# Input parts of later token pairs made ahead, and weights rounded a period ahead, in a fused attention and mixture-of-experts kernel

## The chip, the cores and the metric

The kernel runs on one core of one Trainium2 chip. The metric is the device time of one launch in microseconds; 0.2% of it is 3.75 us. The engines are called PE (TensorE), DVE (VectorE), ACT (ScalarE), POOL (GpSimd) and SP (SyncE, which issues the DMAs).

## The reference

Four batches of eight attention heads over 576 positions, with a learned bias on the scores, give x of 2304 tokens by 512 features. Then every token goes through all eight experts, and the outputs are added with weights from a gate that is normalised over rows and columns eight times:

```python
logits = x @ w_gate
logits = logits - logits.max()
P = np.exp(logits)
for _ in range(8):
    P /= P.sum(1, keepdims=True) + 1e-09
    P /= P.sum(0, keepdims=True) + 1e-09
    P *= N / E
out = np.zeros((N, D), dtype=np.float32)
for e in range(E):
    h = np.maximum(x @ w1[e], 0.0)
    ye = h @ w2[e]
    out += P[:, e:e + 1] * ye
```

with N = 2304 tokens, D = 512, E = 8 experts and F = 1024 hidden units each.

## The kernel before

The first 345 us are attention; from there on the kernel is the expert stage. Tokens are taken in three pairs of blocks of 384 (`TILE_PAIRS` = 3, numbered p = 0 to 2). For each pair the loop goes over 32 periods: eight experts, four pairs of 128 hidden units each. So g, the period, runs from 0 to 95, and p = g // 32. The three pairs use the same weights, loaded again for each.

In a period PE does two things. First **seven products**: x @ w1 for two blocks of tokens and two of hidden units is a 2 by 2 block product, done in seven block products instead of eight (sums and differences of blocks on both sides). Each factor is kept as a rounded high part and the rest, its low part; a product is high by high, low by high and high by low, over two halves of the depth: six matmuls of 384 columns, 42 in all. Then **six tiles**: the second layer of the period before, h @ w2, six matmuls of 512 columns for each of six tiles of 128 tokens, 36 in all. 78 matmuls are one period.

What the other engines do for it in a period, each in the order of its own queue:

- ACT copies the first product out of PSUM (`keep_first`, p1_copy), later the third (`keep_corner`), rounds four blocks of h (`round_hidden`), and rounds the weights of the next period in three parts (`round_weights`: part 0 is raw blocks, 768 wide; part 1 the sums, 1024; part 2 is w2, 1024).
- DVE makes u2, u3 and three corners from the products (`combine`), and h_lo, the low parts of h (`split_hidden`, four). After an expert's last period it adds the six tiles to the output (`add_tile`). In periods 2 to 8 it also does the gate's normalisation; its column totals are small matmuls between PE's tiles.
- POOL makes the low parts of the weights (`split_weights`, three) and the weight sums two periods ahead (`sum_weights`, four). In periods 4 to 7 of a pair it makes the four sums of the next pair's blocks (`sum_factor`), over raw blocks of x that are no longer needed.
- SP loads the weights of a later period when both buffers of the stage allow it.

Everything is ordered by semaphores. PE's product 2 waits for p1_copy, product 3 for u2, product 4 for the corner copy, product 5 for u3, product 6 for the first corner. The weights w1 lie in two buffers, w2 in three. The third part of `round_weights` waits for `h_used`, which counts the periods whose tiles PE has done.

**At the start of a pair** the seven x factors have to be rounded (ACT, `round_factor`, into `x_hi`) and split (`split_factor`, into `x_lo`). There is one `x_hi` and one `x_lo` per factor, so a factor of the new pair can be made only when the last product of the old pair that reads it is done. Factors 0 and 1 and 4 are split on DVE and 2, 3, 5 and 6 on POOL, around the end of the pair's last period and in the first of the new one. In that first period PE doesn't do seven products and then six tiles, but mixes them:

```python
APART = ((), (0, 1), (), (2, 3), (), (4,), (5,))
TOGETHER = ((), (), (), (), (), (), tuple(range(TJ)))
```

Of the kernel before, what the change touches and what calls it, by code (L numbers as in the profile page):

```python
# [13 lines left out]
P = 128  # L14
# [33 lines left out]
APART = ((), (0, 1), (), (2, 3), (), (4,), (5,))  # L48
TOGETHER = ((), (), (), (), (), (), tuple(range(TJ)))
ON_GPSIMD = (2, 3, 5, 6)  # L50
# [34 lines left out]
def bass_attention_moe(nc, qk, v, bias_w, gate_w, expert_w, log_table, inv_psi, identity, pair_select, out):  # L85
    with ExitStack() as ctx:
# [24 lines left out]

        def first_weights(i):
            return [sb(f"w1_{part}{i}", [P, NP, BLOCK], F32R) for part in ("hi", "lo")]
# [16 lines left out]
        x = sb("x", [P, DC, N])  # L130
# [26 lines left out]
        logits_t = sb("logits_t", [P, 2, T])  # L157
# [4 lines left out]
        x_lo_first = sb("x_lo_first", [P, EARLY, 2, T], F32R)  # L162
        p1_copy = sb("p1_copy", [P, T])
        x_lo_rest = sb("x_lo_rest", [P, NP - EARLY, 2, T], F32R)
# [43 lines left out]
        x_split_late = sem("x_split_late")  # L208
# [59 lines left out]
        def x_block(p, half, part):  # L268

            return x[:, 2 * half:2 * half + 2, (2 * p + part) * T:(2 * p + part) * T + T]  # L270

        def x_sum(p, i):
# [4 lines left out]
            return x_block(p - 1, i % 2, i // 2)  # L277

        def x_factor(p, k):

            return (x_block(p, 0, 0), x_sum(p, 1), x_block(p, 1, 0), x_sum(p, 2), x_sum(p, 0), x_sum(p, 3),
                    x_block(p, 1, 1))[k]
# [17 lines left out]
        def tiles_after(g, k):  # L300

            return (APART if 0 < g < ALL and g % PERIODS == 0 else TOGETHER)[k]

        def x_low(k):
            return x_lo_first[:, k] if k < EARLY else x_lo_rest[:, k - EARLY]

        def splits_before(p, k):

            late = [j for j in ON_GPSIMD if j < k]
            if p == 0:  # L310
                return k, 0
            return NP + (NP - len(ON_GPSIMD)) * (p - 1) + k - len(late), len(ON_GPSIMD) * (p - 1) + len(late)

# [119 lines left out]
        def _(pe):  # L433
# [159 lines left out]
            def product(g, k):  # L593
# [3 lines left out]
                if g % PERIODS == 0:  # L597
                    on_vector, on_gpsimd = splits_before(p, k + 1)
                    if p > 0 and k in ON_GPSIMD:
                        pe.wait_ge(x_split_late, on_gpsimd)  # L600
                    else:
                        pe.wait_ge(x_split, on_vector)
# [25 lines left out]
                for c in range(2):  # L628
                    f = slice(c * P, c * P + P)
                    pe.matmul(dst, hi[:, w, f], x_hi[:, k, c, :], start=fresh and c == 0, stop=False,  # L630
                              skip_group_check=not fresh)
                    pe.matmul(dst, hi[:, w, f], x_low(k)[:, c, :], start=False, stop=False,  # L632
                              skip_group_check=not fresh)
                    mm = pe.matmul(dst, lo[:, w, f], x_hi[:, k, c, :], start=False, stop=c == 1,  # L634
# [89 lines left out]
            for g in range(ALL + 1):  # L724
                for k in range(NP):
# [4 lines left out]
                    if g > 0:  # L730
# [8 lines left out]
        def _(act):  # L739
# [77 lines left out]
            def round_weights(g, i):  # L817
# [14 lines left out]
            def round_factor(p, k):  # L832

                if p == 0:
                    act.wait_ge(scores_ready, 2 * (LAST - QC))
                    act.wait_ge(split_done, 2 * X_PIECES)
                    act.wait_ge(scaled, PIECES_0)
                else:
                    act.wait_ge(product_done, NP * (PERIODS * p - 1) + k + 1)
                needed = (0, 2, 0, 3, 1, 4, 0)[k]  # L840
                if needed:
                    act.wait_ge(x_summed, SUMS * p + needed)
                act.activation(x_hi[:, k], x_factor(p, k), ACT.Copy).then_inc(x_rounded, 1)
# [54 lines left out]
            for g in range(ALL):  # L898
                p, at = g // PERIODS, g % PERIODS
                more = g + 1 < ALL  # L900
                after = at == PERIODS - 1 and more
# [10 lines left out]
                if more:  # L912
                    round_weights(g + 1, 0)
# [3 lines left out]
                if after:  # L917
                    round_factor(p + 1, 0)
                if more:
                    round_weights(g + 1, 1)  # L920
                round_hidden(g, 1)
                if after:
                    round_factor(p + 1, 1)
                if more:
                    round_weights(g + 1, 2)
                round_hidden(g, 2)
                round_hidden(g, 3)
                if after:
                    for k in range(2, 5):
                        round_factor(p + 1, k)  # L930
# [3 lines left out]
        def _(dve):  # L934
# [116 lines left out]
            def split_factor(p, k):  # L1051
# [3 lines left out]
                dve.tensor_tensor(x_low(k), x_factor(p, k), x_hi[:, k].bitcast(F32),  # L1055
# [115 lines left out]
            for g in range(ALL):  # L1171
                p, at = g // PERIODS, g % PERIODS
                after = at == PERIODS - 1 and g + 1 < ALL
# [3 lines left out]
                if at == 0 and p > 0:  # L1177
                    split_factor(p, 4)
                    add_tile(g - 1, 0)
                dve.wait_ge(product_done, NP * g + 4)  # L1180
                combine(u3[:], product_bank(g, 1), p1_copy[:], ALU.add)
                if at == 0 and p > 0:
                    add_tile(g - 1, 1)
                    add_tile(g - 1, 2)
# [5 lines left out]
                split_hidden(g, 0)  # L1190
                if after:
                    split_factor(p + 1, 0)
# [3 lines left out]
                combine(corner[:, 3, :], product_bank(g, 0), u2[:], ALU.add)  # L1196
                split_hidden(g, 1)
# [3 lines left out]
                if at > 0:  # L1201
# [173 lines left out]
```

## Time and profile before

| | |
|---|---|
| median of three timed runs | 1874.88 us (1873.86 to 1876.94) |
| the profiled execution | 1876.01 us |
| its span, first to last instruction | 1874.2 us |
| PE busy | 1846.2 us, 99% |
| DVE, ACT, POOL busy | 1298.8, 809.3, 1139.4 us |
| mean granted clock of PE | 0.996 |

The span is the profiled execution without what lies before its first and behind its last instruction (1.8 us). PE is the engine that the others serve; the busy time of the others matters only where PE, or an engine that PE waits for, stands behind it. Matmuls overlap: one of 384 columns lasts 0.33 us and the next starts 0.17 us after it.

### The profile page before, as it was taken

Reading aid. Unit: us, or ns where it says so; the run is one execution under the profiler, and the core shown is the slowest. Engines: PE = TensorE matmul, PEld = TensorE weight load, DVE = VectorE, ACT = ScalarE, POOL = GpSimd, SP = SyncE. Lnnn points to the kernel's source line nnn. Section 1 sums busy time; section 2 is a strip of 40 time slices with the busy share of each in tenths; the row PEclk is TensorE's granted clock in tenths of the full one; section 3 lists DMA queues with packets and bytes.
Section 4 is the critical chain, followed back from the end, with each engine's and each line's share of the span. In section 5 each row is a group of like instructions: output and inputs, shape, how many; then the busy total and the mean of one; then the engine's idle time right before and its main releaser. Section 6 shows DMA issues by size and latency. Waiting matters only on the chain.

```text
span 1874.2 us, 28089 instructions
## 1 busy us (share of the span) xinstructions
PE 1846.2 (99%) x10255; PEld 1600.3 (85%) x10255; DVE 1298.8 (69%) x1838; ACT 809.3 (43%) x1410; POOL 1139.4 (61%) x728
## 2 busy tenths in 40 slices
PE   8999999999999999998999999999989999999999
PEld 4677777788899999997999999999889999999998
DVE  8877777778766666666666666666656666666664
ACT  8776777633333333333333333333433333333331
POOL 0223326467766666668687666666766666666662
PEclk9999999999999999999999999999999999999999
DMA  7753452011111111112112212111121111111110
GB/s 246 220 147 93 124 151 57 33 68 68 68 68 68 68 67 68 68 68 102 51 70 71 71 71 72 70 67 68 68 79 68 68 68 68 68 68 68 68 68 34
DMA packets 44163, 152.57 MB, mean 81 GB/s; under 512 B 9594, under 2 KB 18042, under 8 KB 29710
## 3 DMA queue, kind: packets, MB, share of 16 engines
q1 hardware_dynamic: 44046, 151.04, 24.7%
q8 instruction: 70, 1.15, 0.3%
q14 instruction: 47, 0.39, 0.1%
HBM read 135.69 MB, written 15.34 MB: 81 GB/s over the span
## 4 chain that ended last, share of the span: by engine, by line
PE 90%; DVE 4%; issue 1%; ACT 1%; POOL 0%; DVEq 0%; ACTq 0%; POOLq 0%
PE banks L663 13%; PE banks L664 13%; PE banks L662 13%; PE banks L630 12%; PE banks L634 12%; PE banks L632 12%; PE banks L541 4%; PE banks L502 3%; PE banks L484 3%; PE banks L485 2%; DVE h_lo L1145 2%; PE banks L567 1%; DVE routing L1113 0%; DVE x_lo_first L1055 0%; PE banks L512 0%
## 5 line engine op out<-in xcount | busy, mean ns | idle before, releaser
L1254 POOL TENSOR_TENSOR w_lo<-stage,w_hi 128x1024 fp32r<-128x1024 f32 (+1 forms) x288 | 689.8, 2421 | 460.8 <-ACT w_hi L830 459.6
L1145 DVE SCALAR_TENSOR_TENSOR h_lo<-corner,h_hi 128x384 fp32r<-128x384 f32 x384 | 648.8, 1718 | 0.0
L630 PE MATMUL banks<-x_hi,w_hi 128*128 128x384 f32 x1344 | 453.6, 338 | 13.1 <-DVE u L1139 6.5
L634 PE MATMUL banks<-x_hi,w_lo 128*128 128x384 f32 x1344 | 452.0, 336 | 0.0
L664 PE MATMUL banks<-w_hi,h_lo 128*128 128x512 f32 x1152 | 450.3, 391 | 0.0
L663 PE MATMUL banks<-w_lo,h_hi 128*128 128x512 f32 x1152 | 450.2, 391 | 0.0
L662 PE MATMUL banks<-w_hi,h_hi 128*128 128x512 f32 x1152 | 449.1, 390 | 0.0
L1139 DVE TENSOR_TENSOR u<-p_copy,banks 128x384 f32<-128x384 f32 x192 | 106.3, 554 | 423.0 <-PE banks L634 422.9
L860 ACT ACTIVATE p_copy<-banks 128x384 f32<-128x384 f32 x96 | 47.2, 492 | 710.7 <-PE banks L634 710.7
L830 ACT ACTIVATE w_hi<-stage 128x1024 fp32r<-128x1024 f32 (+1 forms) x288 | 272.1, 975 | 1.1 <-POOL stage L1248 1.1
L630 PEld LDWEIGHTS banks<-x_hi,w_hi 128*128 128x128 f32 x1344 | 253.5, 189 | 21.6 <-DVE u L1139 8.2
L632 PE MATMUL banks<-x_lo_rest,w_hi 128*128 128x384 f32 x768 | 258.0, 336 | 0.0
L664 PEld LDWEIGHTS banks<-w_hi,h_lo 128*128 128x128 f32 x1152 | 216.3, 188 | 45.3
L634 PEld LDWEIGHTS banks<-x_hi,w_lo 128*128 128x128 f32 x1344 | 253.6, 189 | 0.0
L662 PEld LDWEIGHTS banks<-w_hi,h_hi 128*128 128x128 f32 x1152 | 216.6, 188 | 42.5
L663 PEld LDWEIGHTS banks<-w_lo,h_hi 128*128 128x128 f32 x1152 | 216.4, 188 | 42.7
L871 ACT ACTIVATE h_hi<-corner 128x384 fp32r<-128x384 f32 x384 | 196.4, 526 | 77.6 <-DVE corner L1139 74.5
L632 PE MATMUL banks<-x_lo_first,w_hi 128*128 128x384 f32 x576 | 193.5, 336 | 0.0
L1139 DVE TENSOR_TENSOR corner<-u,banks 128x384 f32<-128x384 f32 x288 | 150.5, 546 | 59.5 <-PE banks L634 59.4
L1229 POOL TENSOR_TENSOR qk_hi<-raw,qk_hi 64x1152 fp32r<-64x1152 f32 x15 | 39.9, 2659 | 229.6 <-ACT qk_hi L763 162.2
L794 ACT ACTIVATE probs<-probs,neg_max 128x576 f32<-128x576 f32 (+1 forms) x160 | 123.4, 771 | 79.6 <-DVE neg_max L1012 77.6
L1012 DVE CUSTOM_DVE_ANT_0 probs<-banks,bias 128x576 f32<-128x576 f32 (+1 forms) x160 | 117.8, 752 | 53.8 <-PE banks L485 48.7
(103 smaller groups left out, 2004.2 us busy)
## 6 DMA issues: line engine op xcount, KB each, us to landing
stage<-in_expert_w SPq DMA_DIRECT2D x96, 1024.0 KB, 4.7
raw<-in_qk SPq DMA_DIRECT2D x32, 576.0 KB, 7.2
bias_scratch<-bias_out SPq DMA_DIRECT2D x36, 288.0 KB, 2.7
bias<-bias_scratch SPq DMA_DIRECT2D x16, 288.0 KB, 2.8
v_main<-in_v SPq DMA_DIRECT2D x16, 256.0 KB, 2.7
bias<-bias_scratch SPq DMA_DIRECT2D x16, 256.0 KB, 3.7
out<-total SPq DMA_DIRECT2D x4, 768.0 KB, 3.8
out<-total SPq DMA_DIRECT2D x6, 256.0 KB, 2.0
```

Of the source, the lines that this page charges most:

```text
L630: pe.matmul(dst, hi[:, w, f], x_hi[:, k, c, :], start=fresh and c == 0, stop=False, skip_group_check=not fresh)
L632: pe.matmul(dst, hi[:, w, f], x_low(k)[:, c, :], start=False, stop=False, skip_group_check=not fresh)
L634: mm = pe.matmul(dst, lo[:, w, f], x_hi[:, k, c, :], start=False, stop=c == 1, skip_group_check=not fresh)
L662: pe.matmul(dst, h_hi[:, g % 2, f, tokens], hi[:, f], start=fp == 0 and f == 0, stop=False)
L663: pe.matmul(dst, h_hi[:, g % 2, f, tokens], lo[:, f], start=False, stop=False)
L664: mm = pe.matmul(dst, h_lo[:, g % 2, f, tokens], hi[:, f], start=False, stop=fp == FPAIRS - 1 and f == 1)
L794: act.activation(row, row, ACT.Exp, bias=neg_max[0:rows, 2 * (s % 2) + h:2 * (s % 2) + h + 1], scale=-1.0, accum_out=row_sum[0:rows, slot, ...
L830: act.activation(hi, of, ACT.Copy).then_inc(w_rounded, 1)
L871: act.activation(h_block(h_hi, g, f, part), corner[:, i, :], ACT.Relu).then_inc(h_rounded, 1)
L1139: dve.tensor_tensor(out, other, bank, op).then_inc(combined, 1)
L1145: dve.scalar_tensor_tensor(h_block(h_lo, g, f, part), corner[:, i, :], 0.0, h_block(h_hi, g, f, part).bitcast(F32), ALU.max, ALU.subtract) ...
L1254: pool.tensor_tensor(lo, of, hi.bitcast(F32), ALU.subtract).then_inc(w_split, 1)
```

## The change

1. **High parts of a later pair go to free places** (`high_part`): parts of the memory of x, of the logits and of `x_hi` or `x_lo` places that the pair before has no use for.
2. **Low parts are written over their own raw blocks** (`low_part`), so they need no place of their own. The block sums of pairs 1 and 2 go to other places than before (`x_sum`), and POOL makes them in the order 0, 2, 1, 3.
3. **Factors are made ahead** (`IN_ADVANCE`): at the end of ACT's and DVE's work of a period, one factor. For pair 1 factor 0 in period 11 and 1 in period 13, for pair 2 factors 0 to 5 in its predecessor's periods 9, 10, 11, 13, 14 and 15, which are g = 41, 42, 43, 45, 46 and 47. The rest, factors 2 to 6 of pair 1 and 6 of pair 2, are made in the last period before the pair, g = 31 and g = 63, at fixed places between the other work. All low parts are now made on DVE, none on POOL.
4. **One order everywhere**: `APART` is gone, PE does seven products and then six tiles in every period.
5. **Weights are rounded a period earlier**: in period g ACT rounded those of g+1 between the `round_hidden` steps; now it rounds those of g+2 behind them, at the end of its work of period g. Period 0 does both. Where the period's w2 place was last read by an expert's last period, the wait is on `y_done` instead of `h_used`: the same matmul's end.

```diff
-ON_GPSIMD = (2, 3, 5, 6)
+IN_ADVANCE = {1: {11: 0, 13: 1}, 2: {9: 0, 10: 1, 11: 2, 13: 3, 14: 4, 15: 5}}
...
+        def high_part(p, k):
+
+            if p == 0:
+                return x_hi[:, k]
+            spare = x_block(0, 1, 1, x_r)
+            if p == 1:
+                return (spare, logits_r[:], x_hi[:, 0], first_low(0), x_hi[:, 1], first_low(1),
+                        x_hi[:, 2])[k]
+            return (x_hi[:, 3], x_hi[:, 4], x_hi[:, 5], x_hi[:, 6], first_low(5), first_low(6), spare)[k]
+
+        def low_part(p, k):
+
+            return first_low(k) if p == 0 else x_factor(p, k, rounded=True)
...
-                        for j in tiles_after(g, k):
-                            second_layer(g - 1, j)
-                            side_work(g, j)
+                if g > 0:
+                    for j in range(TJ):
+                        second_layer(g - 1, j)
+                        side_work(g, j)
...
+                elif g > 2 and (g - 2) % FPAIRS == 0:
+                    act.wait_ge(y_done, TJ * ((g - 2) // FPAIRS))
                 elif g > 2:
                     act.wait_ge(h_used, g - 2)
...
                 keep_first(g)
-                if at == 0 and p > 0:
-                    for k in range(5, NP):
-                        round_factor(p, k)
+                if after == 1:
+                    for k in range(2, 4):
+                        round_factor(1, k)
+                elif after == 2:
+                    round_factor(2, 6)
                 keep_corner(g)
...
-                if more:
-                    round_weights(g + 1, 1)
+                if g == 0:
+                    round_weights(1, 1)
                 round_hidden(g, 1)
...
                 round_hidden(g, 3)
-                if after:
-                    for k in range(2, 5):
-                        round_factor(p + 1, k)
+                if after == 1:
+                    round_factor(1, 6)
+                if g + 2 < ALL:
+                    for i in range(NW):
+                        round_weights(g + 2, i)
+                if at in IN_ADVANCE.get(p + 1, {}):
+                    round_factor(p + 1, IN_ADVANCE[p + 1][at])
...
                 for j in range(3, TJ):
                     read_side(g, j)
                     add_tile(g - 1, j)
+                if after == 1:
+                    for k in range(4, NP):
+                        split_factor(1, k)
+                elif after == 2:
+                    split_factor(2, 6)
+                if at in IN_ADVANCE.get(p + 1, {}):
+                    split_factor(p + 1, IN_ADVANCE[p + 1][at])
```

**The end of period 11 on ACT.** Before, with w_hi the rounded weights, p_copy the first copy of the next period and corner, h_hi what belongs to the hidden blocks:

```order
L877 ACTIVATE corner<-banks 128x384 [waits h_split,product_done]
L871 ACTIVATE h_hi<-corner 128x384 [waits h_used,corner_kept]
L830 ACTIVATE w_hi<-stage 128x768 [waits product_done,w_in0]
L830 ACTIVATE w_hi<-stage 128x1024 [waits w_summed]
L871 ACTIVATE h_hi<-corner 128x384 [waits combined]
L830 ACTIVATE w_hi<-stage 128x1024 [waits h_used]
L871 ACTIVATE h_hi<-corner 128x384 [waits combined] x2
L860 ACTIVATE p_copy<-banks 128x384 [waits combined,product_done]
```

Now, the same place (x_r is the memory of x, written as a rounded part):

```order
L895 ACTIVATE corner<-banks 128x384 [waits h_split,product_done]
L889 ACTIVATE h_hi<-corner 128x384 [waits h_used,corner_kept]
L889 ACTIVATE h_hi<-corner 128x384 [waits combined] x3
L842 ACTIVATE w_hi<-stage 128x768 [waits product_done,w_in1]
L842 ACTIVATE w_hi<-stage 128x1024 [waits w_summed]
L842 ACTIVATE w_hi<-stage 128x1024 [waits h_used]
L861 ACTIVATE x_r<-x 128x2x384 [waits x_split,x_summed]
L878 ACTIVATE p_copy<-banks 128x384 [waits combined,product_done]
```

The three weight parts moved behind the hidden blocks and are those of one period later; the factor stands between w2's part and the next period's p_copy.

**The end of period 11 on DVE**, before and then now:

```order
L1139 TENSOR_TENSOR corner<-u,banks 128x384 [waits product_done] x2
L1145 SCALAR_TENSOR_TENSOR h_lo<-corner,h_hi 128x384 [waits h_rounded] x3
L1139 TENSOR_TENSOR u<-p_copy,banks 128x384 [waits p1_kept,product_done]
L1139 TENSOR_TENSOR u<-p_copy,banks 128x384 [waits product_done]
L1139 TENSOR_TENSOR corner<-u,banks 128x384 [waits combined,product_done]
```

```order
L1164 TENSOR_TENSOR corner<-u,banks 128x384 [waits product_done] x2
L1170 SCALAR_TENSOR_TENSOR h_lo<-corner,h_hi 128x384 [waits h_rounded] x3
L1080 TENSOR_TENSOR x_r<-x,x_r 128x2x384 [waits x_summed,x_rounded]
L1164 TENSOR_TENSOR u<-p_copy,banks 128x384 [waits p1_kept,product_done]
L1164 TENSOR_TENSOR u<-p_copy,banks 128x384 [waits product_done]
L1164 TENSOR_TENSOR corner<-u,banks 128x384 [waits combined,product_done]
```

The split of the factor stands between the last h_lo and the next period's u2, and waits for ACT's rounding.

**The end of period 0 and the start of period 1 on ACT**, before and then now:

```order
L871 ACTIVATE h_hi<-corner 128x384 [waits combined]
L830 ACTIVATE w_hi<-stage 128x1024
L871 ACTIVATE h_hi<-corner 128x384 [waits combined] x2
L884 ACTIVATE logits_t<-banks 128x384 [waits logit_done]
L884 ACTIVATE logits_t<-banks 40x384
L860 ACTIVATE p_copy<-banks 128x384 [waits combined,product_done]
```

```order
L889 ACTIVATE h_hi<-corner 128x384 [waits combined] x2
L842 ACTIVATE w_hi<-stage 128x768 [waits product_done,w_in0]
L842 ACTIVATE w_hi<-stage 128x1024 [waits w_summed]
L842 ACTIVATE w_hi<-stage 128x1024
L902 ACTIVATE logits_t<-banks 128x384 [waits logit_done]
L902 ACTIVATE logits_t<-banks 40x384
L878 ACTIVATE p_copy<-banks 128x384 [waits combined,product_done]
```

The three parts of period 2's weights now stand ahead of the copies of the logits, which PE turns in period 1 before its product 2.

## Rows read from the trace of the kernel before

**Rows 1.** The page: busy us, share of the span, instructions, of each engine.

```profile
PE 1846.2 (99%) x10255; PEld 1600.3 (85%) x10255; DVE 1298.8 (69%) x1838; ACT 809.3 (43%) x1410; POOL 1139.4 (61%) x728
```

**Rows 2.** Waits of PE, whole span: us in total, times, longest.

```profile
PE banks L630 <- DVE u L1139: 6.5, 4, 2.8
...
PE banks L630 <- DVE x_lo_first L1055: 4.5, 2, 2.3
...
PE banks L630 <- POOL x_lo_rest L1258: 1.6, 2, 0.8
```

**Rows 3.** Stretches of two periods: us, busy us (instructions), PE's granted clock, DMA.

```profile
666.03:697.05 31.02, 31.02 (x157) 1.00 0.19 69
852.11:891.49 39.38, 33.56 (x157) 0.96 0.30 111
1356.69:1397.49 40.80, 35.02 (x157) 0.92 0.29 105
```

**Rows 4.** Timeline around the start of an ordinary period: start, us, engine, line.

```profile
665.82 0.39 PE L664 MATMUL banks<-w_hi,h_lo 128*128 128x512 f32 x1
666.04 0.33 PE L630 MATMUL banks<-x_hi,w_hi 128*128 128x384 f32 x1
...
667.31 0.49 ACT L860 ACTIVATE p_copy<-banks 128x384 f32<-128x384 f32 x1 [7.74 <-PE banks L634]
...
668.15 0.33 PE L630 MATMUL banks<-x_hi,w_hi 128*128 128x384 f32 x1
...
668.35 0.55 DVE L1139 TENSOR_TENSOR u<-p_copy,banks 128x384 f32<-128x384 f32 x1 [3.91 <-PE banks L634]
...
669.19 0.33 PE L630 MATMUL banks<-x_hi,w_hi 128*128 128x384 f32 x1
...
669.39 0.49 ACT L877 ACTIVATE corner<-banks 128x384 f32<-128x384 f32 x1 [1.59 <-PE banks L634]
```

**Rows 5.** Timeline: what roundings and splits take, alone and beside each other.

```profile
841.89 4.54 POOL L1254 TENSOR_TENSOR w_lo<-stage,w_hi 128x768 fp32r<-128x768 f32 x2 [4.77 <-ACT w_hi L830]
...
842.38 1.04 ACT L830 ACTIVATE w_hi<-stage 128x1024 fp32r<-128x1024 f32 x1
...
843.33 0.51 ACT L871 ACTIVATE h_hi<-corner 128x384 fp32r<-128x384 f32 x1
...
844.09 3.16 DVE L1055 TENSOR_TENSOR x_lo_first<-x,x_hi 128x768 fp32r<-128x768 f32 x1
...
853.71 1.04 POOL L1243 TENSOR_TENSOR stage<-stage 128x256 f32<-128x256 f32 x1
853.77 1.57 ACT L843 ACTIVATE x_hi<-x 128x768 fp32r<-128x768 f32 x2
854.08 1.48 DVE L1055 TENSOR_TENSOR x_lo_first<-x,x_hi 128x768 fp32r<-128x768 f32 x1
...
882.87 2.40 POOL L1254 TENSOR_TENSOR w_lo<-stage,w_hi 128x1024 fp32r<-128x1024 f32 x1 [1.58 <-ACT w_hi L830]
...
347.67 2.69 DVE L1055 TENSOR_TENSOR x_lo_rest<-total,x_hi 128x768 fp32r<-128x768 f32 x3
```

**Rows 6.** Timeline of the start-up, periods 0 and 1.

```profile
364.92 0.86 ACT L884 ACTIVATE logits_t<-banks 128x384 f32<-128x384 f32 x2 [4.16 <-PE banks L681]
...
366.95 0.73 POOL L1248 TENSOR_TENSOR stage<-stage 128x256 f32<-128x256 f32 x1
...
366.99 0.80 PE L692 MATMUL banks<-ident,logits_t 128*128 128x128 f32 x6
```

**Rows 7.** A stretch as in rows 3, behind the second idle at pair 1.

```profile
878.61:882.02 3.41, 3.41 (x12) 0.50 1.03 357
```

**Rows 8.** Waits of PE in periods 6 to 8, columns as in rows 2.

```profile
PE banks L630 <- DVE u L1139: 1.0, 2, 0.6
```

**Rows 9.** Timeline of DVE at the start of PE's period 6.

```profile
446.31 1.52 DVE L1113 SCALAR_TENSOR_TENSOR routing<-routing,col_sum 128x144 f32<-128x144 f32 x1
```

More of the change, by code:

```diff
@@ L110, in bass_attention_moe, with twice @@
         total = sb("total", [P, TJ, DM])
+        def twice(name, shape):
+            with ExitStack() as scope:
+                as_f32 = sb(name, shape, F32, scope)
+            return as_f32, sb(f"{name}_r", shape, F32R)
         def first_weights(i):
@@ L128, in bass_attention_moe @@
             hidden = sb("hidden", [P, ROUND * GROUPS, S], F32, inner)
-        x = sb("x", [P, DC, N])
+        x, x_r = twice("x", [P, DC, N])
         with ExitStack() as early:
@@ L265, in columns_free, with x_block, x_sum @@
             return {0: before + PV_DONE[0], HALF // P: before + PV_DONE[1]}.get(s % QC)
-        def x_block(p, half, part):
-            return x[:, 2 * half:2 * half + 2, (2 * p + part) * T:(2 * p + part) * T + T]
-        def x_sum(p, i):
+        def x_block(p, half, part, of=x):
+            return of[:, 2 * half:2 * half + 2, (2 * p + part) * T:(2 * p + part) * T + T]
+        def x_sum(p, i, rounded=False):
             if p == 0:
@@ L276, in x_sum, with x_factor @@
                     "p (c t) -> p c t", c=2)
[L277 to L282, printed above, removed]
+            if i == 1:
+                return x_block(p, 0, 1, x_r if rounded else x)
+            if p == 1:
+                return x_block(0, i // 3, i // 2 % 2 if i < 3 else 0, x_r if rounded else x)
+            at = {0: 2, 2: 3, 3: 4}[i]
+            if rounded:
+                return first_low(at)
+            return x_sum_first[:, at] if at < EARLY else x_sum_rest[:, at - EARLY]
+        def x_factor(p, k, rounded=False):
+            if k in (0, 2, 6):
+                return x_block(p, k // 2 % 2 if k < 6 else 1, k // 6, x_r if rounded else x)
+            return x_sum(p, {1: 1, 3: 2, 4: 0, 5: 3}[k], rounded)
         def weight_part(g, i):
@@ L597, in product @@
                 if g % PERIODS == 0:
[L598 to L602, printed above, removed]
+                    pe.wait_ge(x_split, NP * p + k + 1)
                 if k == 0:
@@ L837, in round_factor @@
                     act.wait_ge(scaled, PIECES_0)
-                else:
[L839 to L843, printed above, removed]
+                    needed = (0, 2, 0, 3, 1, 4, 0)[k]
+                    if needed:
+                        act.wait_ge(x_summed, needed)
+                else:
+                    act.wait_ge(x_summed, SUMS * (p + 1))
+                if p == 1:
+                    act.wait_ge(x_split, NP)
+                    if k > 1:
+                        act.wait_ge(product_done, NP * (PERIODS - 1) + k // 2)
+                elif p == 2:
+                    act.wait_ge(product_done, NP * PERIODS if k < 6 else NP * (2 * PERIODS - 1) + 1)
+                act.activation(high_part(p, k), x_factor(p, k), ACT.Copy).then_inc(x_rounded, 1)
             for s in range(STEPS):
@@ L900, in _ @@
                 more = g + 1 < ALL
-                after = at == PERIODS - 1 and more
+                after = p + 1 if at == PERIODS - 1 and more else None
                 if g == 1:
@@ L911, in _ @@
                 round_hidden(g, 0)
-                if more:
-                    round_weights(g + 1, 0)
+                if after == 1:
+                    for k in range(4, 6):
+                        round_factor(1, k)
+                if g == 0:
+                    round_weights(1, 0)
                 if g == 2:
@@ L1172, in _ @@
                 p, at = g // PERIODS, g % PERIODS
-                after = at == PERIODS - 1 and g + 1 < ALL
+                after = p + 1 if at == PERIODS - 1 and g + 1 < ALL else None
                 dve.wait_ge(product_done, NP * g + 2)
@@ L1189, in _ @@
                     largest_logit()
-                split_hidden(g, 0)
-                if after:
-                    split_factor(p + 1, 0)
+                if after == 1:
+                    split_factor(1, 3)
+                else:
+                    split_hidden(g, 0)
                 dve.wait_ge(product_done, NP * g + 6)
@@ L1196, in _ @@
                 combine(corner[:, 3, :], product_bank(g, 0), u2[:], ALU.add)
+                if after == 1:
+                    split_hidden(g, 0)
                 split_hidden(g, 1)
```

93 lines of the change are left out of this document (32 added, 61 removed).

## The prediction

> **What bounds the kernel now.** I read the page first: TensorE (PE) is busy 99% of the span [rows 1], so only its idle time, or time at the low clock, can be won. The table of waits of PE says where it idles: in the expert stage nearly all of it stands before line 630, the first matmul of a product, for u, for a low part of x made on VectorE and for one made on GpSimd [rows 2]. The stretches say when. In the middle of the stage 157 matmuls take 31.02 us, two periods of 15.51. The same 157 take 39.38 us where pair 1 of the token blocks begins and 40.80 us where pair 2 begins [rows 3]: 8.36 and 9.78, together 18.1 us more. Part of it is clock: the granted mean is 0.96 and 0.92 there, so PE ran at the lower of its two levels (1.2 instead of 2.4 GHz) for about 3.4 and 6.8 us, each time just after it had idled. Everything else of the stage already runs at 15.51.
>
> An ordinary period, with T = 666.04 its first matmul, is the clock for the rest [rows 4]. The last matmul of the tiles before ends at T+0.17. ScalarE (ACT) starts p1_copy at T+1.27 and ends it at T+1.76; PE needs it for product 2 at T+2.11. VectorE (DVE) makes u2 from T+2.31 to T+2.86; PE needs it for product 3 at T+3.15. Slack: 0.35 and 0.29 us. DVE has nothing else to do just then.
>
> **1. The boundaries, removed.** Before, the factors of the next pair are rounded and split around the first two periods of the pair, and product and tile groups alternate there to wait less. Now pair 1 has two factors made in periods 11 and 13 and five in period 31; pair 2 has six in periods 41 to 47 and one in period 63. I walked period 31, the fullest: two roundings (0.83 each, 0.74 apart [rows 5]) fit in the 1.59 us that ACT idles between the p1_copy and corner copies [rows 4]; the split after u2 meets a GpSimd operation and ends about T+4.6, u3 then ends about 5.1, and product 5 wants it at 5.2; the last three splits end about 1.5 us into the next period, before its u2. I take the whole 18.1 back, with 0 to 1.5 us of remaining stall for the range: **-18.1**.
>
> **2. Advance parts, added in eight periods.** The order on ACT is now: second-layer weights w2 of period g+2, then the factor, then p1_copy of g+1. w2's rounding waits for h_used, that is for the last matmul of the tiles, so it can't start before T+0.2 of the next period. Behind it everything on ACT is late. Step by step: w2's copy T+0.22 to 1.26 (1.04 long, the next one starts 0.95 after it); factor T+1.17 to 2.00; p1_copy T+1.91 to 2.40 instead of 1.76. PE restarts some 0.06 after what it waits for, so product 2 starts at 2.46, 0.35 late.
>
> DVE is worse off. Its split_factor stands ahead of u2 of g+1 in the queue and waits for the factor's rounding, T+2.05. At that moment GpSimd (POOL) is splitting the w2 part that ACT released at T+1.26: it runs from about T+1.36 for 2.40 us [rows 5] to T+3.76. The rows show what a DVE subtraction of two tiles in SBUF does when POOL is at work: the one of 3.16 us ends at 847.25, 0.82 after POOL's pair of operations (846.43); the one of 1.48 ends at 855.56, 0.81 after POOL's (854.75); without POOL three in a row take 2.69, 0.9 each [rows 5]. So x_lo ends at 3.76+0.82 = T+4.58, u2 runs 4.50 to 5.05, product 3 starts at 5.10 instead of 3.15, and the first matmul after a stall costs 0.1 more. That is 2.05 us a time, product 2's lateness inside it. Eight times: **+16.4**. Bounds: 0.5 each if the split ran at its lone 0.95 (x_lo 3.0, u2 3.5, product 3 at 3.6), 4 in all; above, 2.05 each plus a clock drop each time (part 4).
>
> The Trainium skill (SBUF — State Buffer, Who interferes with whom) says a VectorE instruction with two SBUF inputs and a GpSimd one that reads SBUF take the shared ports in turn, each for its whole length. If it were instead a common slowing, the 3.16 us of the worst row would be the length (x_lo to T+5.2, product 3 at 5.75, 2.7 us a time) and the sum some 21 us; by the page's rule it is the 16.4. The trace's two endings at +0.81 and +0.82 agree with the page.
>
> **3. Start-up, added.** Period 0 now ends on ACT with the weights of period 2, ahead of the copies of the logits. The rounding of the sums waits for POOL's fourth sum, which ends at 367.68 [rows 6]. Then 0.05 + 0.95 + 0.95, so the logits copies start at 369.63 instead of 364.92, take 0.86, and PE's transposes start at about 370.55 instead of 366.99: 3.6 us with the restart. p1_copy of period 1 follows at 370.9 and is covered by the 0.80 us of transposes. The earlier work this buys is not needed. **+3.6**, bounds 3 to 4.5.
>
> **4. The clock.** Three of the idles in rows 3 (2.8, 2.7 and one of the two of 2.3 [rows 2]) were followed by a stretch at half clock, the other 2.3 and both of 0.8 by none; 12 matmuls filled 3.41 us [rows 7], where 0.173 each makes 2.1, so a drop costs up to 1.3 to 1.7, I take 1.5. The start-up idle of 3.5 us should cause one: **+1.5**. The eight stalls idle PE for about 1.6 us after 0.3: nearer to the 2.3 that did it once in two than to 0.8. I take one in four: **+3**, bounds 0 and 12.
>
> **5. Rounding a period ahead, all periods.** ACT's w2 copy lets p1_copy start at T+1.17, and its input is there at T+1.27: nothing on the path. Weights are then split 12 us or more before their product, instead of just behind it: also nothing, since PE never waited for them. POOL's subtractions move to T+1.4 to 3.8 and T+9.5 to 14, away from u2's neighbours: the DVE chain of the routing cost 1.0 us of PE idle in periods 6 to 8 [rows 8], part of it because line 1113 took 1.52 beside POOL's sum of x [rows 9]. 0.6 of it may go. I give **-0.6**, bounds -1.6 to +2, for its totals could also be late for PE's side matmuls.
>
> **6. Factors written over raw blocks, the sums order, the uniform tile order** change no count of matmuls and no size; hidden, 0. The tiles of the pair's first period now wait for nothing but what every expert change has.
>
> **Sum**, on the profiled span 1874.2: -18.1 + 16.4 + 3.6 + 1.5 + 3.0 - 0.6 = **+5.8**. That execution took 1876.01 with its surroundings, so 1881.8; against the median of the three timed runs, 1874.88, it is **1880.7 us**.
>
> **Rivals.**
> (a) *The clock holds* through the eight stalls. For it: each idle is shorter than any that was followed by a drop. Then +2.8: 1877.7, within 0.2% (3.75 us, about what this measurement can tell from no change).
> (b) *The advance splits are cheap*: faster. If DVE gets its second input while POOL is at work, or POOL's w2 split is over by T+2.1, each stall is 0.5 and the boundaries' gain stays. -18.1 + 4 + 5.1 - 0.6 = -9.6: **1865.3**. It decides once a stall is under 1.2 us (8 x 1.2 = 9.6). Against it: three rows on which DVE waited POOL out.
> (c) *p1_copy late in every period*: ACT has 0.1 us of free time ahead of it and PE 0.35 behind. If waking from h_used took 0.5 instead of 0.05, each of some 90 periods would lose about 0.1: +9, 1890. Against it: PE's other releases of ACT take 0.05.
> (d) *Neither boundary is really gone*: if period 31's splits overran by 2 us and drew a clock drop, +3.5, 1884; inside the range.
>
> **How the numbers follow.** Forecast with (d) 0.58; (a) and like cancellations 0.22; (b) 0.14 and 0.02 more for smaller gains; (c) 0.04. Slower 0.62, same 0.22, faster 0.16. The range leaves out (b) and the far end of (c): from 1871 (half of the advance stalls short) to 1890 (a drop at each stall).
>
> **What would show it.** Waits of PE before the product line: about eight of 1.5 us for DVE's u and eight of 0.3 for ACT's p_copy, in periods 12, 14, 42 to 44 and 46 to 48; periods 32, 33, 64 and 65 at 15.5; an idle of 3.5 us before the transposes of the logits; each x_lo of an advance period starting about T+2.05 and ending 0.8 after POOL's w2 split. Wrong would be: x_lo of 0.95 there, a p_copy after T+1.3 in ordinary periods, or PE waiting again in periods 31 to 33.

## The result and the profile after

The changed kernel takes 1878.55 us (median of 13 runs, 1875.33 to 1879.69) against 1874.78 for the kernel before (13 runs, 1872.77 to 1876.94): a ratio of 1.0019, 95% interval 1.0011 to 1.0028. It is slower by 3.8 us or 0.2%: the interval leaves out 1, and the difference is at the bound of what the prediction counts as a change (3.75 us). The forecast was 1880.7. The profiled execution took 1878.12 us, its span is 1876.3.

First the page of the changed kernel, the row that answers to [rows 1]:

```profile
PE 1844.5 (98%) x10255; PEld 1595.6 (85%) x10255; DVE 978.4 (52%) x1846; ACT 830.1 (44%) x1410; POOL 1059.5 (56%) x720
```

DVE does eight operations more and is busy 320 us less. PE waited for little of that time (6.5 and 4.5 us in all before [rows 2]), but it says that the engines now meet differently; the last section has the numbers.

The waits of PE over the whole span, against [rows 2] (us in total, times, longest):

```profile
PE banks L640 <- DVE u L1164: 10.5, 8, 1.3
...
PE banks L702 <- ACT logits_t L902: 3.0, 1, 3.0
...
PE banks L640 <- ACT p_copy L878: 1.2, 8, 0.2
PE banks L720 <- DVE col_part L1127: 0.6, 2, 0.3
```

All waits for a low part of x are gone. In their place stand eight for u, eight for p_copy, one for the logits.

Stretches, all engines (us, then busy us and instructions of PE, PEld, DVE, ACT, POOL; PE's granted clock, DMA): periods 32 and 33, 64 and 65, then period 12 alone, then period 1.

```profile
859.81:890.82 31.01, 31.01 (x157) 28.12 (x156) 18.17 (x25) 11.78 (x18) 19.64 (x15) 1.00 0.32 119
...
1368.20:1399.22 31.02, 31.02 (x157) 28.12 (x156) 17.06 (x24) 11.89 (x18) 19.19 (x14) 1.00 0.32 119
...
545.60:563.14 17.54, 16.07 (x79) 13.99 (x78) 12.73 (x14) 6.45 (x10) 10.44 (x7) 1.00 0.18 61
...
364.00:387.20 23.20, 19.89 (x89) 17.22 (x87) 7.62 (x14) 8.16 (x16) 16.27 (x13) 0.85 0.26 91
```

The first two answer to the second and third of [rows 3]: 39.38 and 40.80 us are now 31.01 and 31.02, the length of any two periods. Period 12 takes 17.54 instead of 15.51, and so do 14, 42 to 44 and 46 to 48. Period 1 takes 23.20 (17.39 before, at full clock); its mean clock of 0.85 says that PE ran at 1.2 GHz for a part of it. That part is one stretch of 6.83 us, and it began while PE still stood idle (its transposes of the logits start at 369.39, the copies that they wait for at 368.86):

```profile
366.95 2.00 ACT L842 ACTIVATE w_hi<-stage 128x1024 fp32r<-128x1024 f32 x2 [6.21 <-POOL stage L1274]
368.86 0.84 ACT L902 ACTIVATE logits_t<-banks 128x384 f32<-128x384 f32 x2
...
369.39 1.37 PE L702 MATMUL banks<-ident,logits_t 128*128 128x128 f32 x6 [3.00 <-ACT logits_t L902]
```

and as a stretch of PE (us, busy us, granted clock, DMA):

```profile
368.44:375.27 6.83, 5.88 (x20) 0.50 0.12 23
```

The timeline of period 12, T = 545.59, is the prediction's part 2 in rows (start, us, engine, line):

```profile
545.59 0.33 PE L640 MATMUL banks<-x_hi,w_hi 128*128 128x384 f32 x1
545.79 1.06 ACT L842 ACTIVATE w_hi<-stage 128x1024 fp32r<-128x1024 f32 x1 [5.40 <-PE banks L674]
...
546.76 0.83 ACT L861 ACTIVATE x_r<-x 128x768 fp32r<-128x768 f32 x1
546.93 2.39 POOL L1280 TENSOR_TENSOR w_lo<-stage,w_hi 128x1024 fp32r<-128x1024 f32 x1 [3.15 <-ACT w_hi L842]
...
547.50 0.47 ACT L878 ACTIVATE p_copy<-banks 128x384 f32<-128x384 f32 x1
547.62 2.51 DVE L1080 TENSOR_TENSOR x_r<-x,x_r 128x768 fp32r<-128x768 f32 x1 [8.07 <-ACT x_r L861]
548.02 0.44 PE L640 MATMUL banks<-x_hi,w_hi 128*128 128x384 f32 x1 [0.15 <-ACT p_copy L878]
...
550.05 0.54 DVE L1164 TENSOR_TENSOR u<-p_copy,banks 128x384 f32<-128x384 f32 x1
550.65 0.45 PE L640 MATMUL banks<-x_hi,w_hi 128*128 128x384 f32 x1 [1.32 <-DVE u L1164]
```

Read it downwards. ACT stood idle 5.40 us until PE's last tile let it round w2's part, at T+0.20. Behind that come the factor (T+1.17) and p_copy (T+1.91, ordinary T+1.27). DVE had stood idle 8.07 us for the factor. Its split starts at T+2.03, while POOL's split runs to 549.32, and it ends at 550.13, 0.81 behind it. Then u2, then PE at T+5.06 instead of T+3.15.

### The profile page after: what moved, and what is told of

It is laid out like the page before. It is cut to its first block, busy times and chain, and to the rows that moved or that the text cites. A ratio compares the mean times of both kernels' runs of the same rounds, so it can differ in the third digit from the quotient of the medians.

```text
span 1876.3 us, 28109 instructions
## 1 busy us (share of the span) xinstructions
PE 1844.5 (98%) x10255; PEld 1595.6 (85%) x10255; DVE 978.4 (52%) x1846; ACT 830.1 (44%) x1410; POOL 1059.5 (56%) x720
## 4 chain that ended last, share of the span: by engine, by line
PE 91%; DVE 2%; issue 2%; ACT 1%; POOL 1%; DVEq 0%; ACTq 0%; POOLq 0%
PE banks L673 14%; PE banks L674 14%; PE banks L672 14%; PE banks L640 12%; PE banks L644 12%; PE banks L642 12%; PE banks L555 4%; PE banks L516 3%; PE banks L498 3%; PE banks L499 2%; PE banks L581 1%; PE banks L526 0%; DVE probs L1035 0%; POOL w_lo L1280 0%; DVE u L1164 0%
## 5 line engine op out<-in xcount | busy, mean ns | idle before, releaser
L1280 POOL TENSOR_TENSOR w_lo<-stage,w_hi 128x1024 fp32r<-128x1024 f32 (+1 forms) x288 | 645.5, 2255 | 524.7 <-ACT w_hi L842 523.4
L640 PE MATMUL banks<-x_hi,w_hi 128*128 128x384 f32 x896 | 302.8, 338 | 4.2 <-DVE u L1164 2.6
L644 PE MATMUL banks<-x_hi,w_lo 128*128 128x384 f32 x896 | 300.9, 336 | 0.0
L1170 DVE SCALAR_TENSOR_TENSOR h_lo<-corner,h_hi 128x384 fp32r<-128x384 f32 x384 | 295.0, 798 | 0.0
L642 PE MATMUL banks<-x_r,w_hi 128*128 128x384 f32 x704 | 235.7, 335 | 0.0
L1164 DVE TENSOR_TENSOR corner<-u,banks 128x384 f32<-128x384 f32 x288 | 159.3, 554 | 94.0 <-PE banks L644 92.4
L640 PEld LDWEIGHTS banks<-x_hi,w_hi 128*128 128x128 f32 x896 | 168.9, 188 | 11.0 <-ACT p_copy L878 3.8
L644 PEld LDWEIGHTS banks<-x_hi,w_lo 128*128 128x128 f32 x896 | 168.9, 188 | 0.0
L642 PEld LDWEIGHTS banks<-x_r,w_hi 128*128 128x128 f32 x704 | 132.2, 188 | 2.5
L642 PE MATMUL banks<-x_lo_rest_r,w_hi 128*128 128x384 f32 x384 | 128.8, 335 | 0.0
```

The source lines that it names most:

```text
L640: pe.matmul(dst, hi[:, w, f], high_part(p, k)[:, c, :], start=fresh and c == 0, stop=False, skip_group_check=not fresh)
L642: pe.matmul(dst, hi[:, w, f], low_part(p, k)[:, c, :], start=False, stop=False, skip_group_check=not fresh)
L644: mm = pe.matmul(dst, lo[:, w, f], high_part(p, k)[:, c, :], start=False, stop=c == 1, skip_group_check=not fresh)
L1164: dve.tensor_tensor(out, other, bank, op).then_inc(combined, 1)
L1170: dve.scalar_tensor_tensor(h_block(h_lo, g, f, part), corner[:, i, :], 0.0, h_block(h_hi, g, f, part).bitcast(F32), ALU.max, ALU.subtract) ...
L1280: pool.tensor_tensor(lo, of, hi.bitcast(F32), ALU.subtract).then_inc(w_split, 1)
```

## The experiments

Every kernel is compared with the kernel before on the same chip. That one had 1874.78, 1873.94 and 1874.4 us in the three sets below.

The changed kernel was not run again in them; it stands at its 1878.55.

### The first set: each cost removed, and the two halves of the change

**e1**, the factor ahead of the weights on ACT:

```diff
+                if at in IN_ADVANCE.get(p + 1, {}):
+                    round_factor(p + 1, IN_ADVANCE[p + 1][at])
                 if g + 2 < ALL:
                     for i in range(NW):
                         round_weights(g + 2, i)
-                if at in IN_ADVANCE.get(p + 1, {}):
-                    round_factor(p + 1, IN_ADVANCE[p + 1][at])
```

> The changed kernel, but on ACT the advance factor is rounded ahead of the weights of period g+2 instead of behind them. My theory (the factor waits behind w2's part, which waits for PE's last tile, and DVE's split, ahead of u2, waits with it): all eight stalls of 2.0 us go, 16.2 us off, some 1862.3. Rival (the stalls come from one more instruction on ACT and DVE in such a period, wherever it stands, or from DVE and POOL meeting): at least the split still costs 0.5 to 2 a time, 1866 to 1878. The start-up idle of 3.0 us stays in both.

Measured: 1863.12 us, ratio 0.9936 (0.9920 to 0.9951). All eight stalls are gone, the periods take 15.51. The end of period 11 in its timeline:

```profile
539.47 0.83 ACT L861 ACTIVATE x_r<-x 128x768 fp32r<-128x768 f32 x1
540.20 1.78 ACT L842 ACTIVATE w_hi<-stage 128x768 fp32r<-128x768 f32 x2
540.33 0.96 DVE L1080 TENSOR_TENSOR x_r<-x,x_r 128x768 fp32r<-128x768 f32 x1
541.17 1.84 POOL L1280 TENSOR_TENSOR w_lo<-stage,w_hi 128x768 fp32r<-128x768 f32 x1 [3.19 <-ACT w_hi L842]
```

The same two instructions, in time in which both engines were idle, cost nothing. That rules out the rival by which the additional work itself costs. Moving two lines is worth 15.4 us. The start-up idle of 3.0 us stays, as expected.

**e2**, the weights of period 2 at their old places, behind the logits:

```diff
-                if g == 0:
-                    round_weights(1, 0)
+                if g < 2:
+                    round_weights(g + 1, 0)
...
-                if g + 2 < ALL:
+                if 0 < g < ALL - 2:
                     for i in range(NW):
                         round_weights(g + 2, i)
```

(and the same for parts 1 and 2)

> The changed kernel, but the weights of period 2 are rounded in period 1 at their old places, behind the copies of the logits. My theory (the logits wait behind the rounding of the sums, that stall costs 3.7 and the low clock behind it another 2.1): 5.8 us off, 1872.8, and no stretch at half clock in the expert stage. Rival (the clock falls for another reason, or the wait only moves to the first product of period 2): 2 to 4 us off.

Measured: 1873.42 us (10 runs), ratio 0.9990 (0.9981 to 1.0000). The wait for the logits is gone, period 1 takes 17.41 us, and no stretch at half clock is left in the expert stage. That is 5.1 us off, 0.7 less than expected. In the profiles the expert stage up to its last period shows the whole 5.8 (1502.5 us in the changed kernel, 1496.7 here). The rest lies outside it: this execution had a stretch of 3.41 us at half clock at 61.8 us, in the attention, and the profile of the changed kernel had none there.

**e3**, both edits:

> Both edits. If the costs are separate they add: 16.2 + 5.8 = 22 off the changed kernel, 1856.5, which is 18.2 under the kernel before. Rival (one idle feeds the other, or the low clock turns up elsewhere): 1858 to 1862.

Measured: 1857.09 us, ratio 0.9905 (0.9890 to 0.9920), 21.5 off the changed kernel, against 15.4 + 5.1 = 20.5 for the two edits alone: within 1 us the two costs add. PE's waits in the expert stage are down to these:

```profile
PE banks L720 <- DVE col_part L1127: 0.6, 2, 0.3
...
PE banks L640 <- DVE top L1114: 0.3, 1, 0.3
```

It was measured again in the third set (e9 below) and is the fastest version of the study.

**e7**, the parts made ahead without rounding the weights ahead:

```diff
-                if g == 0:
-                    round_weights(1, 0)
+                if more:
+                    round_weights(g + 1, 0)
...
-                if g + 2 < ALL:
-                    for i in range(NW):
-                        round_weights(g + 2, i)
                 if at in IN_ADVANCE.get(p + 1, {}):
                     round_factor(p + 1, IN_ADVANCE[p + 1][at])
```

> The changed kernel with the weights rounded for the next period at the old places: only the parts made ahead, low parts over raw blocks, and one order. My theory (rounding a period ahead is what costs, the rest is a pure gain of 18.1, early periods as before): 1856.7, the advance factors rounded near the ninth us of a period and no stall in periods 12 to 48. Rival (period 31 with five factors and three weight parts on ACT doesn't fit, or POOL's splits late in the period push DVE's splits over u2): 1860 to 1866, with stalls in periods 31 to 33.

Measured: 1860.18 us, ratio 0.9919 (0.9906 to 0.9933), 3.5 above my figure and inside the rival's range. No stall in periods 12 to 48, as expected, but one in period 32. Its timeline there:

```profile
853.16 1.49 DVE L1077 TENSOR_TENSOR x_r<-x,x_hi 128x768 fp32r<-128x768 f32 x1
...
854.57 1.49 DVE L1077 TENSOR_TENSOR x_r<-x,x_lo_first_r 128x768 fp32r<-128x768 f32 x1
...
855.98 1.49 DVE L1077 TENSOR_TENSOR x_r<-x,x_hi 128x768 fp32r<-128x768 f32 x1
...
857.39 0.54 DVE L1161 TENSOR_TENSOR u<-p_copy,banks 128x384 f32<-128x384 f32 x1
...
858.08 0.41 PE L640 MATMUL banks<-x_lo_first_r,w_hi 128*128 128x384 f32 x1 [1.40 <-DVE u L1161]
```

The last three splits for pair 1 each meet one of POOL's sums, take 1.49 instead of 0.95 and push u2 back: period 32 takes 1.6 us more. Of the other 1.9 us, 1.2 can be put down to the figure that I started from: it took 18.1 off the median, though the 18.1 is read from an execution 1.2 above it (see the next section). The early periods 2 to 8 take 113.3 us together, as before (113.3), where the changed kernel has 111.8.

### The second set: ACT's part, POOL's part, and rounding ahead alone

**e4**, DVE's advance split behind u2, ACT as in the changed kernel:

```diff
                 combine(u2[:], product_bank(g, 1), p1_copy[:], ALU.add)
+                if at - 1 in IN_ADVANCE.get(p + 1, {}):
+                    split_factor(p + 1, IN_ADVANCE[p + 1][at - 1])
...
-                if at in IN_ADVANCE.get(p + 1, {}):
-                    split_factor(p + 1, IN_ADVANCE[p + 1][at])
```

> The changed kernel, ACT as it is (factor behind w2's part), but DVE splits the advance factor behind u2 of the next period instead of ahead of it. It tells ACT's part of the stall from DVE's. My theory: ACT's lateness alone is 0.32 us a time at product 2 and stays, the 1.7 us at product 3 go: 8 x 1.7 = 13.6 off, 1865.0; x_lo still ends 0.82 behind POOL's w2 split, near T+4.6, u3 wants to start at T+4.7 and isn't late. Rival (u2 is late because p1_copy is, not because of the split): nothing changes, 1878.5.

Measured: 1865.90 us, ratio 0.9954 (0.9937 to 0.9971). The eight periods take 15.96 us, 0.45 over the ordinary ones where I had 0.32: the first matmul after a wait starts its successor 0.1 late. In the expert stage's periods PE waits only for p_copy, and no longer for u:

```profile
PE banks L640 <- ACT p_copy L878: 1.2, 8, 0.2
```

In the timeline of its period 12 the split now runs after u2 and still ends 0.82 behind POOL's operation (547.06+2.39 = 549.45; 548.67+1.60 = 550.27):

```profile
547.06 2.39 POOL L1280 TENSOR_TENSOR w_lo<-stage,w_hi 128x1024 fp32r<-128x1024 f32 x1 [3.15 <-ACT w_hi L842]
...
548.19 0.56 DVE L1164 TENSOR_TENSOR u<-p_copy,banks 128x384 f32<-128x384 f32 x1 [8.51 <-ACT p_copy L878]
548.67 1.60 DVE L1080 TENSOR_TENSOR x_r<-x,x_r 128x768 fp32r<-128x768 f32 x1
```

So of each stall of 2.03 us, 0.45 is ACT's and 1.6 is DVE's.

**e5**, POOL splits w2's part only behind DVE's advance split:

```diff
                 for i in range(NW):
+                    if i == 2 and at - 1 in IN_ADVANCE.get(p + 1, {}):
+                        pool.wait_ge(x_split, NP * (p + 1) + IN_ADVANCE[p + 1][at - 1] + 1)
                     if g + 1 < ALL:
                         split_weights(g + 1, i)
```

> The changed kernel, but in the eight periods POOL splits w2's part only when DVE's advance split is done. It tells the wait on ACT from the meeting with POOL. My theory (DVE stands until POOL's operation is over): x_lo then takes 0.95 from T+2.05, u2 ends at 3.5, product 3 starts at about 3.6 instead of 5.1, the stalls are 0.5 each: 8 x 1.5 = 12 off, 1866.5. Rival (the split waits for its input or runs at its contended length for another reason): x_lo stays above 2 us and 0 to 3 us come off.

Measured: 1865.64 us, ratio 0.9954 (0.9937 to 0.9971). Its period 12 takes 16.00:

```profile
547.14 0.96 DVE L1080 TENSOR_TENSOR x_r<-x,x_r 128x768 fp32r<-128x768 f32 x1 [8.07 <-ACT x_r L861]
...
548.02 0.55 DVE L1164 TENSOR_TENSOR u<-p_copy,banks 128x384 f32<-128x384 f32 x1
548.18 2.40 POOL L1280 TENSOR_TENSOR w_lo<-stage,w_hi 128x1024 fp32r<-128x1024 f32 x1 [4.88 <-DVE x_r L1080]
```

With POOL out of the way the split takes 0.96 from the same start, T+2. POOL's place is all that differs, so the 1.5 us that the split took longer in the changed kernel come from POOL's operation in progress. DVE waiting for ACT costs little by itself; what costs is that it then meets POOL.

**e6**, the kernel before with the weights rounded a period ahead and nothing else:

```diff
-                if more:
-                    round_weights(g + 1, 0)
+                if g == 0:
+                    round_weights(1, 0)
...
                 if after:
                     for k in range(2, 5):
                         round_factor(p + 1, k)
+                if g + 2 < ALL:
+                    for i in range(NW):
+                        round_weights(g + 2, i)
```

(with the wait on `y_done`, as in the change)

> The kernel before with the weights rounded a period ahead and nothing else of the change: factors, places and the mixed order of before. My theory: +5.8 at the start-up, -1.4 in the early periods, 0 in the middle; and at the pair boundaries ACT's rounding of the sums now waits for POOL's sums, which stand behind two factor splits there, with p1_copy behind it: 0 to 6 us a boundary. 1879 to 1891. Rival (rounding ahead is what removed the boundary stalls): 1861 to 1870.

Measured: 1865.81 us, ratio 0.9956 (0.9939 to 0.9972). My theory missed by 13 us and more, and the rival's range holds it. The start-up cost (period 1: 22.2 us) and the early gain (periods 2 to 8: 111.8) are there as expected. But the boundaries, which I had getting worse, fall from 8.4 and 9.8 us to 2.3 each: periods 32 and 64 take 15.66, 33 and 65 take 17.66. DVE's rows in period 31 show why. In e6, around the splits of factors 0 and 1:

```profile
845.95 0.95 DVE L1060 TENSOR_TENSOR x_lo_first<-x,x_hi 128x768 fp32r<-128x768 f32 x1
...
847.75 1.49 DVE L1150 SCALAR_TENSOR_TENSOR h_lo<-corner,h_hi 128x384 fp32r<-128x384 f32 x3
849.15 0.95 DVE L1060 TENSOR_TENSOR x_lo_first<-x,x_hi 128x768 fp32r<-128x768 f32 x1
```

In the kernel before the same two splits take 3.16 and 1.48 [rows 5], and the three h_lo between them

```profile
848.10 6.06 DVE L1145 SCALAR_TENSOR_TENSOR h_lo<-corner,h_hi 128x384 fp32r<-128x384 f32 x3
```

With POOL's weight splits out of the way DVE has both low parts ready at 850.10, 5.0 us before period 32 begins (855.09). In the kernel before the second was ready 3.4 us into period 32 (855.56, its first matmul at 852.12), and PE stood idle 2.3 us until then. Its other long idle there, 2.8 us for u2 of period 33, stood behind three h_lo that took 4.28; here they take 2.80. What is left is the wait that I expected there, only smaller; in period 33:

```profile
871.48 0.94 POOL L1253 TENSOR_TENSOR stage<-stage 128x256 f32<-128x256 f32 x1
872.45 2.00 ACT L832 ACTIVATE w_hi<-stage 128x1024 fp32r<-128x1024 f32 x2 [1.04 <-POOL stage L1253]
...
874.36 0.47 ACT L862 ACTIVATE p_copy<-banks 128x384 f32<-128x384 f32 x1
874.88 0.19 PEld L630 LDWEIGHTS banks<-x_hi,w_hi 128*128 128x128 f32 x1 [2.21 <-ACT p_copy L862]
```

### The third set: what the parts made ahead add

**e8**, e6 with the start-up edit of e2, and **e9**, e3 once more:

```diff
-                if g == 0:
+                if g < 2:
-                    round_weights(1, 0)
+                    round_weights(g + 1, 0)
...
-                if g + 2 < ALL:
+                if 0 < g < ALL - 2:
```

> The kernel before with the weights rounded a period ahead, except those of period 2, which keep their old places behind the copies of the logits. If the start-up cost is the same thing here as in the changed kernel, period 1 falls from 22.2 to 17.4: 1861.0, with 2.1 us of stall left at each pair boundary. Rival (the boundary stalls come back without the start-up wait): 1865 or more.

> The kernel with both edits once more, on the same chip as the one above: 1857.1 if the first measurement holds. The parts made ahead are then worth what rounding ahead leaves of the boundaries, 2 x 2.3 = 4.6 less the noise of the clock: 3.5 to 4.6 under the one above. Rival (the two sets of edits cover the same stalls entirely): no difference.

Measured: 1863.03 us for e8 (ratio 0.9934, 0.9921 to 0.9948) and 1857.10 for e9 (0.9906, 0.9891 to 0.9921). e9 repeats e3 to 0.01 us. e8 is 2.0 above what I expected. Its period 1 fell to 17.4 as foreseen, but in its profile the wait of 1.9 us in period 33 was followed by a stretch at half clock, and that period took 19.25 us instead of 17.66:

```profile
871.29 0.45 PE L630 MATMUL banks<-x_hi,w_hi 128*128 128x384 f32 x1 [1.90 <-ACT p_copy L862]
```

and as a stretch, columns as above:

```profile
871.90:875.31 3.41, 3.41 (x13) 3.41 (x12) 0.30 (x1) 1.02 (x2) 3.41 (x2) 0.51 0.94 315
```

The one run of e8 with a mean clock of 1.000 took 1860.87, as expected; the other four, at 0.998, 1862.69 to 1863.44. So the 2.0 us are the clock. In the profile 1.6 of them are this stretch; a second one of 3.41 us, at 63.0 us, is in the attention and has nothing to do with the edits. The parts made ahead are worth 5.9 us on top of rounding ahead by the medians. By the two executions without a stretch at half clock, 1860.87 here and 1856.36 of e3, they are worth 4.5, which is the 2 x 2.3 = 4.6 that the profile shows as stall; the rest is the clock.

## Why the prediction was right, and where it wasn't

The sum of the prediction beside the profiles (periods by the starts of their first matmuls):

| term | predicted | profile after | 
|---|---|---|
| 1, the boundaries | -18.1 | -18.1 |
| 2, advance parts | +16.4 | +16.2 (eight of 2.02 to 2.04) |
| 3 and the start-up's share of 4 | +5.1 | +5.8 |
| 4, the clock in the eight periods | +3.0 | 0 |
| 5, the early periods | -0.6 | -1.4 |
| sum | +5.8 | +2.5 |

The spans differ by 2.1: the expert stage also began 0.7 earlier in this execution, and its last period and what follows took 0.3 longer. The execution of the kernel before had a stretch at half clock in the attention, at 62.8 us, and this one had none there.

**Part 1** was right as a size: 31.01 and 31.02 us, and period 31 overran by 0.02. But it gave the whole gain to the parts made ahead and rounding ahead nothing, in part 5. The experiments show that each half takes back most of it alone: e7 16.5 of the 18.1 us, e6 13.5. That step was wrong as an account of causes. Part 5 only asked whether PE waits for weights. It didn't ask what DVE could do once POOL's splits had moved out of its way: in e6 its boundary splits take 0.95 each instead of 3.16 and 1.48. The forecast didn't depend on it, because the change makes both.

**Part 2** was right to 0.03 us a stall, and its working holds step by step: e5 (the meeting with POOL, 1.5 us), e4 (ACT's share), e1 (all of it is the order). For rival (b), cheap advance splits, the experiments show what it would have needed: e5 is that case made by hand, and it lands at 1865.6, where (b) said 1865.3. Its stalls are the 0.5 us that (b) had; that the totals agree to 0.3 is in part luck, since (b) rests on the same sum as the forecast. The case against it named three rows; those of two splits, both in rows 5, show DVE's work ending a fixed time behind POOL's.

**Part 3** was right in mechanism, and two sizes in it were off. PE's transposes came 3.2 us later, not 3.6: the copies of the logits started where the working had them, but PE went on 0.53 us behind the start of the first of the two and didn't wait for both (0.84). The low clock cost 2.6 where I had 1.5: the transposes then took 1.37 instead of 0.80, and the fifteen matmuls behind them, 0.32 apart, lost 2.1. The stretch lasted 6.83 us here and in e1, where it began before the idle of 3.0 us was over. In e4, e5 and e6 it began 1.7 to 1.9 us behind the idle and lasted 3.41, and the start-up cost 4.8 us instead of 5.8:

```profile
372.47:375.88 3.41, 3.41 (x13) 0.50 0.19 24
```

(e4, columns as above; its transposes start at 370.55)

**Part 4** is the step that was mis-sized. I took one drop of the clock in four for the eight stalls; there was none in the profile, nor in that of e2, which has the same eight. Rival (a), the clock holds, forecast 1877.7 and is what the profiles show. In each of the eight periods PE waits 0.15 and then 1.32 us, and the granted clock stays at 1.00. Of the other twelve runs only the mean clock is known. Four have 0.997, but so has the profile of e1, which has no such stall and a stretch in the attention instead.

**Part 5** was right in sign. In the early periods both late u's of before are gone, and two side matmuls wait 0.3 us each for the column sums: the totals late for PE, as the bounds had it. The remark ahead of the parts that everything but the boundaries runs at 15.51 doesn't hold for these periods: 2 to 8 took 113.3 us together before, 4.7 more than seven of 15.51.

**Rival (c)** is priced too high in the prediction. ACT 0.45 us later, less its 0.1 of free time, uses up PE's 0.35 exactly, so nothing is left to lose but the 0.1 of a restart at most. In no profile here does PE wait for p_copy in an ordinary period.

One more thing made the sum a little too kind to the change: it took back 18.1 us from one execution of the kernel before whose clock had dropped three times at the boundaries. That execution was 1.2 us above the median of 13. e3, which has neither cost, is 17.7 under the kernel before and not 18.1 + 1.4 = 19.5. Weighed against the median, the boundaries are worth 16.3 (17.7 - 1.4) to 16.9 (18.1 - 1.2). So that the forecast came within 2.2 us is partly luck: 3.0 too much for the clock in the eight periods and 0.8 too little gain in the early ones stand against 0.7 too little at the start-up and a boundary gain that was 1.2 or more too large.

What stays open: whether an idle drops the clock. Over all kernels here the idle of 3.0 us before the transposes did in every profile that has it (one of the changed kernel's 13 runs, the 1875.33, has a mean clock of 1.000, so not always), those of 2.3 and 1.9 sometimes did, and 1.3 never. An idle of 1.9 to 2.0 us in the attention, at 60 to 62 us, has a drop behind it in six profiles (the kernel before, e1, e2, e4, e8, e9) and none in those of the changed kernel and e6. The case shows no more.

## What to carry to other kernels

- An instruction placed in an engine's queue behind one that waits for another engine's last piece of work inherits that wait, and so does everything behind it and whoever waits for its result. Here two instructions of 0.8 and 1.0 us, in engines that were idle half of the time, cost 2 us each time, and nothing once they stood three lines earlier. Before placing "free" work, ask what the instruction ahead of it in the same queue waits for.
- Where a change does two things that aim at the same stall, try each alone before adding the costs of both. Either half gave 8 to 15 us; both, as first built, lost 4; both with their order mended give 17.7.
- The price of two engines meeting can be read from rows where they met before. The prediction had two such rows and priced each stall to 0.03 us with them. In all eleven profiles, from the end of the attention on, 80 of DVE's 128x768 subtractions started while a POOL instruction was running; every one ended 0.81 or 0.82 us after that instruction did. The other 127 took 0.94 to 0.96.

## What the runs showed of the hardware

VectorE and GpSimd met much less once the weight splits had moved by a few microseconds. The same 384 h_lo operations in the kernel before, then in the changed one (busy us, mean ns of one):

```profile
L1145 DVE SCALAR_TENSOR_TENSOR h_lo<-corner,h_hi 128x384 fp32r<-128x384 f32 x384 | 648.8, 1718 | 0.0
```

```profile
L1170 DVE SCALAR_TENSOR_TENSOR h_lo<-corner,h_hi 128x384 fp32r<-128x384 f32 x384 | 295.0, 798 | 0.0
```

It is the rounding ahead that does it. With it alone (e6), and then with only the parts made ahead (e7):

```profile
L1150 DVE SCALAR_TENSOR_TENSOR h_lo<-corner,h_hi 128x384 fp32r<-128x384 f32 x384 | 295.8, 801 | 0.0
```

```profile
L1167 DVE SCALAR_TENSOR_TENSOR h_lo<-corner,h_hi 128x384 fp32r<-128x384 f32 x384 | 655.7, 1735 | 0.0
```

More than half of DVE's busy time for them in the kernel before was waiting for POOL, counted as busy. There, 356 of the 384 ended 0.41 or 0.42 us behind the POOL instruction that was running when they started; in the changed kernel 66 do, and the 318 that started with POOL idle took 0.54 or 0.55. POOL's splits of 1024 columns fell from 2707 to 2451 ns with it. A sum with one operand in PSUM isn't touched: all 192 u's, u2 among them, took 0.54 to 0.56 us in every kernel, and in the changed one 186 of them ran beside a POOL instruction. And DVE's busy share of 69% in the kernel before, which looked like an engine two thirds full, was really 52% of work at most.
